# First expert's tokens taken in by tiles of 128, and the first product of each later expert at the end of the loop round before

## The reference

```python
order = np.argsort(-(x @ w_gate).flatten())
for idx in order:                       # a token goes to the first expert with room
    tok, e = int(idx) // E, int(idx) % E
    if assigned[tok] >= 0 or counts[e] >= cap: continue
    assigned[tok] = e; counts[e] += 1
for e in range(E):                      # 384 tokens each
    h = np.maximum(x[assigned == e] @ w1[e], 0.0)      # 384 -> 1024
    out[assigned == e] = h @ w2[e]                     # 1024 -> 384
```

## Time and profile before

| | us |
|---|---|
| median of 3 runs | 1127.56 |
| runs | 1123.82 to 1131.34 |
| profiled execution | 1126.02 |
| its span | 1124.3 |

### The profile page before, as it was taken

The page is one execution under the profiler, slowest core; times in us unless marked ns, Lnnn a source line. Parts: engine busy times, 40 slices in busy tenths (PEclk is TensorE's granted clock), DMA queues, the critical chain, the costliest instruction groups (busy, mean ns, idle before and its releaser), DMA issues.

```text
span 1124.3 us, 36434 instructions
## 1 busy us (share of the span) xinstructions
PE 1066.0 (95%) x14142; PEld 980.6 (87%) x14142; DVE 811.9 (72%) x1807; ACT 507.6 (45%) x955; POOL 441.4 (39%) x473
## 2 busy tenths in 40 slices
PE   4799999999999829899999999999999999999998
PEld 2588888888888718899999999999999999999998
DVE  6889999999998888856856865865865864874222
ACT  7767777777776333224224324323323323313322
POOL 6556566655556328513313313403403402502501
PEclk9999999999999959999999999999999999999999
DMA  6424443344443252030030030030030030030000
GB/s 134 85 61 91 91 90 80 78 88 91 91 91 80 69 176 96 30 134 2 21 129 5 21 121 14 21 115 20 21 112 22 21 112 22 14 119 21 15 8 22
DMA packets 163640, 73.99 MB, mean 66 GB/s; under 512 B 140016, under 2 KB 158192, under 8 KB 163568
## 3 DMA queue, kind: packets, MB, share of 16 engines
q1 hardware_dynamic: 160496, 63.73, 21.5%
q0 software_dynamic: 3072, 9.44, 2.6%
HBM read 63.71 MB, written 9.44 MB: 65 GB/s over the span
## 4 chain that ended last, share of the span: by engine, by line
PE 59%; DVE 3%; issue 1%; DMA 1%; ACT 0%; POOL 0%; SPq 0%; DVEq 0%; ACTq 0%; POOLq 0%
PE tb L2269 27%; PE acc L1885 8%; PE acc L1887 7%; PE acc L1886 7%; PE tb L1885 2%; PE tb L1887 2%; PE tb L1886 2%; PE ps_r L1789 1%; DVE slot L153 1%; DMA w1s<-in_moe_w 1%; DVE thr L146 0%; PE tb L1868 0%; PE tb L2222 0%; PE tb L2226 0%; PE tb L2223 0%
## 5 line engine op out<-in xcount | busy, mean ns | idle before, releaser
L2080 ACT CAST ab_high<-ab 128x384 fp32r<-128x384 f32 x95 | 48.8, 514 | 222.1 <-DVE ab L2165 222.1
L2165 DVE TENSOR_TENSOR ab<-tb,a_sb 128x384 f32<-128x384 f32 x95 | 52.9, 557 | 98.6 <-PE tb L2269 92.1
L1934 POOL TENSOR_TENSOR w_low<-w1s,w_high 128x384 fp32r<-128x384 f32 x64 | 65.6, 1035 | 144.3 <-ACT w_high L2019 144.3
L1858 POOL DMA_INDIRECT xg<-x_rows,tok_next x24 | 25.7, 1069 | 212.7 <-issue 210.0
L2269 PE MATMUL tb<-x_high,wb_high 128*128 128x384 f32 x288 | 99.9, 347 | 0.0
L1885 PE MATMUL acc<-wo_high,ab_high 128*128 128x384 f32 x288 | 98.5, 342 | 0.1
L2070 ACT COPY a_sb<-tb 128x384 f32<-128x384 f32 x96 | 46.1, 480 | 114.6 <-PE tb L2269 114.6
L1887 PE MATMUL acc<-wo_high,ab_low 128*128 128x384 f32 x288 | 97.5, 339 | 0.0
L2269 PE MATMUL tb<-x_high,wa_high 128*128 128x384 f32 x288 | 97.4, 338 | 0.0
L1886 PE MATMUL acc<-wo_low,ab_high 128*128 128x384 f32 x288 | 97.3, 338 | 0.0
L2269 PE MATMUL tb<-x_high,wb_low 128*128 128x384 f32 x288 | 97.0, 337 | 0.0
(11 more groups left out here) (382 smaller groups left out, 3020.4 us busy)
## 6 DMA issues: line engine op xcount, KB each, us to landing
w1s<-in_moe_w SPq DMA_DIRECT2D x8, 1536.0 KB, 6.3
w2s<-in_moe_w SPq DMA_DIRECT2D x8, 1152.0 KB, 9.4
a_re_in<-in_a_re SPq DMA_DIRECT2D x30, 192.0 KB, 2.9
a_im_in<-in_a_im SPq DMA_DIRECT2D x30, 192.0 KB, 3.7
qk<-in_q SPq DMA_DIRECT2D x24, 192.0 KB, 2.7
qk<-in_k SPq DMA_DIRECT2D x24, 192.0 KB, 3.4
vv<-in_v SPq DMA_DIRECT2D x48, 96.0 KB, 2.9
x_rows<-ysb SPq DMA_DIRECT2D x24, 192.0 KB, 3.1
```

The source lines that it names most:

```text
L1934: nc.gpsimd.tensor_tensor(w1p[1][:, f % NW1, :, :], w1_tile(f), w1p[0][:, f % NW1, :, :].bitcast(F32), ALU.subtract).then_inc(s["w1_low"], 1)
L2080: nc.scalar.copy(abp[0][:, f % 2, :], ab[:, f % 2, :]).then_inc(s["ab_high"], 1)
L2165: nc.vector.tensor_tensor(ab[:, f % 2, :], tb[(2 * f + 1) % 4][:, 0:CAP], a_sb[:, f % 2, :], ALU.mult).then_inc(s["ab_made"], 1)
```

## The change

For the first expert, each tile of tokens is turned into a bank of its own (all three k beside each other), its high part is made by one copy and its low part by one subtraction, and hidden(0) is made tile by tile: `tile_high(i)`, six products of 128 columns, and `tile_low(i)`, three of them. The filling product between tiles 1 and 2 and the one behind are gone. ScalarE makes w1's third high part between tiles 0 and 1. VectorE makes the three low parts ahead of the two comparisons (the generator `second_start` is stopped in between). SyncE waits for the first tile instead of the last before it loads w2. For all later experts hidden(0) is issued as `hidden_first(p + 1)` at the end of round p instead of at the top of round p + 1. `ROUTE_LAYERS` begins with 1 instead of 0, so that the first 12 counting products of a round stand behind hidden(1); the layers are numbered as before, hidden(0) being 0.

```diff
-BETWEEN_TILES = (2, 2, 1)
+BETWEEN_TILES = 2
...
-ROUTE_LAYERS = (0, 5, 9, 13)
+ROUTE_LAYERS = (1, 5, 9, 13)
...
         if first:
-            sp.wait_ge(x_gathered[TT - 1], 16)
+            sp.wait_ge(x_gathered[0], 16)
         sp.dma_start(w2s[:, 0:2, :], rows_of(w2)[:, 0:2, :]).then_inc(m_sem["w2_gathered"], 16)
...
+    of_tile = lambda i: x_banks[i][:, 0:HD].rearrange("p (k t) -> p k t", k=KT)
+
+    def turn_tile(pe, i):
+        pe.wait_ge(x_gathered[i], after_moves("x_gathered", 0))
+        for k in range(KT):
+            mm = nc.tensor.transpose(of_tile(i)[:, k, :], xg[:, i, k * P:(k + 1) * P], ident[:])
+        mm.then_inc(s["x_turned"], 1)
+
+    def split_tile_high(act, i):
+        act.wait_ge(s["x_turned"], after("x_turned", 0, i + 1))
+        nc.scalar.copy(x2[0][:, :, of_tokens(i)], of_tile(i)).then_inc(s["x_high"], 1)
+
+    def split_tile_low(dve, i):
+        dve.wait_ge(s["x_high"], after("x_high", 0, i + 1))
+        nc.vector.tensor_tensor(x2[1][:, :, of_tokens(i)], of_tile(i), x2[0][:, :, of_tokens(i)].bitcast(F32), ALU.subtract
+                                ).then_inc(s["x_low"], 1)
...
             w1_high(0, 0)
             w1_high(0, 1)
-            split_x_high(act, 0)
+            split_tile_high(act, 0)
             w1_high(0, 2)
+            split_tile_high(act, 1)
+            split_tile_high(act, 2)
             w2_high(0, 0)
             w2_high(0, 1)
...
-            for _ in route_start(dve, 1, ...):
-                pass
-            split_x_low(dve, 0)
+            second_start = route_start(dve, 1, ...)
+            next(second_start)
+            for i in range(TT):
+                split_tile_low(dve, i)
+            next(second_start)
...
+            def hidden_open(p):
+                pe.wait_ge(s["ab_made"], after("ab_made", p, FT2, back=1))
+                pe.wait_ge(s["w1_low"], after("w1_low", p, 1))
+                return tb[2][:, 0:CAP], [w[:, 0, :, :] for w in w1p]
+
+            def tile_high(i):
+                bank, (high, low) = hidden_open(0)
+                pe.wait_ge(s["x_high"], after("x_high", 0, i + 1))
+                for k in range(KT):
+                    for w in (high, low):
+                        nc.tensor.matmul(bank[:, of_tokens(i)], w[:, k, :], x2[0][:, k, of_tokens(i)],
+                                         start=(i == k == 0 and w is high), stop=False, skip_group_check=True)
+
+            def tile_low(i):
+                ...
+                pe.wait_ge(s["x_low"], after("x_low", 0, i + 1))
+                for k in range(KT):
+                    mm = nc.tensor.matmul(bank[:, of_tokens(i)], high[:, k, :], x2[1][:, k, of_tokens(i)],
+                                          start=False, stop=(i == TT - 1 and k == KT - 1), skip_group_check=True)
+                return mm
...
             keep_running(WARM_UP)
-            for i, products in enumerate(BETWEEN_TILES):
-                turn_x(pe, 0, (i,))
-                keep_running(products)
+            turn_tile(pe, 0)
+            keep_running(BETWEEN_TILES)
+            turn_tile(pe, 1)
+            tile_high(0)
+            turn_tile(pe, 2)
+            tile_high(1)
+            tile_high(2)
+            for i in range(TT):
+                mm = tile_low(i)
+            mm.then_inc(s["h_summed"], 1)
...
-                layers = [(hidden, 0)]
+                layers = []
...
-                for n, (product_of, f) in enumerate(layers):
+                for n, (product_of, f) in enumerate(layers, 1):
...
                 if not last:
                     add_out(FT2 - 1)
+                    hidden_first(pe.snap(p + 1))
```

More of the change, by code:

```diff
@@ L2129, in _ @@
             in_bank = lambda bank, n: bank[:, n * E * G:(n + 1) * E * G].rearrange("p (e g) -> p e g", e=E)
-            for _ in route_start(dve, 1, scores=in_bank(acc[1], 0), masked=in_bank(acc[0], 0), same=in_bank(acc[0], 1),
-                                 best_again=acc[1][:, E * G:E * G + G]):
-                pass
-            split_x_low(dve, 0)
+            second_start = route_start(dve, 1, scores=in_bank(acc[1], 0), masked=in_bank(acc[0], 0), same=in_bank(acc[0], 1),
+                                       best_again=acc[1][:, E * G:E * G + G])
+            next(second_start)
+            for i in range(TT):
+                split_tile_low(dve, i)
+            next(second_start)
             def expert(p, last):
@@ new lines, in hidden_first @@
+            def hidden_first(p):
+                bank, (high, low) = hidden_open(p)
+                for k in range(KT):
+                    pe.wait_ge(s["x_high"], after("x_high", p, k + 1))
+                    nc.tensor.matmul(bank, high[:, k, :], x2[0][:, k, :], start=(k == 0), stop=False)
+                    nc.tensor.matmul(bank, low[:, k, :], x2[0][:, k, :], start=False, stop=False)
+                for k in range(KT):
+                    pe.wait_ge(s["x_low"], after("x_low", p, k + 1))
+                    mm = nc.tensor.matmul(bank, high[:, k, :], x2[1][:, k, :], start=False, stop=(k == KT - 1))
+                mm.then_inc(s["h_summed"], 1)
@@ L2208, in expert @@
+            keep_running(WARM_UP)
+            turn_tile(pe, 0)
[7 more added lines that the diff above has]
+                mm = tile_low(i)
+            mm.then_inc(s["h_summed"], 1)
             def expert(p, last):
@@ L2218, in hidden @@
                     high, low = (w[:, f % NW1, :, :] for w in w1p)
[L2219 to L2230, removed]
+                    for k in range(KT):
+                        mm = three(bank, [high[:, k, :], low[:, k, :]], [x[:, k, :] for x in x2], k == 0, k == KT - 1)
                     mm.then_inc(s["h_summed"], 1)
```

## The result

The changed kernel is slower: 1136.98 us against 1129.28 (medians of 7 runs each), a ratio of 1.0068 with a 95% interval of 1.005 to 1.0085. The forecast was +6.6 us on 1127.6; measured are +7.7 on medians that lie 1.7 higher. The profiled execution of the changed kernel took 1137.52 us with a span of 1135.8, 11.5 more than the span of before. That difference is not all the change's: the first filling product starts at 420.31 before and at 424.62 after, and up to there the two programs do the same. So 4.3 us of the 11.5 had come before the changed part begins, and every time of the entry is counted here from the first filling product. Of the 7.2 that are left, 6.9 come in the six rounds of the loop and 0.2 in the first expert (103.57 us from the first filling product to the end of the second expert's h0, 103.35 before).

A forecast was written before the change was run, and what follows sets the result against it. From the second expert on, TensorE's queue was taken as the bound (busy 86.00 of 86.00 us a round). A loop loss of 7.0 less an entry gain of 0.4 made +6.6 on 1127.6: 1134.2 us, range 1127.0 to 1138.0.

The forecast's parts named there:

- The loop: Rounds of experts 1 to 6: reply read 0.52 us later, s1 1.18 later, 7.0 us lost in all.
- the row at 450.53: First expert before: thr starts 0.10 us ahead of GpSimd yet takes 1.16; taken as the model for the loop.
- thr would lose: Loop: thr waits for GpSimd's operation in all six rounds, 1134.2 us in all, chance 0.50.
- Branch of the loop at another place: End of each round: h0 ahead of the loop's branch costs nothing, bound 0.5 us a round.
- Narrow products: First expert's entry: products of 128 columns take 0.11 us each, bounded from above by 0.173.
- Gather beside the w2 stream: First expert's entry: w2 loading beside the gather of tile 2 costs 0.3 us, bounds nothing and 3.3.
- Entry: First expert: s1 0.7 us sooner, less 0.3 for the gather, gain 0.4; bounds gain 0.7, loss 3.
- The stall between 460 and 470: First expert: TensorE's stall of 1.77 us stays, since the chains between engines all shift alike.
- rival C: First expert: stall between 460 and 470 goes, with its low clock, 2.8 us gained, 1126.4 in all; chance 0.12.

The follow-up runs named there:

- count_only: The kernel before with only the first entry of ROUTE_LAYERS changed from 0 to 1: 1135.01 us, ratio 1.006 to before.
- count_back: The changed kernel with the first entry of ROUTE_LAYERS back at 0, counting products ahead of hidden(1): 1129.95 us, ratio 1.0014 to before.
- thr_free: The changed kernel with thr in the loop reading its ramp from a copy in PSUM instead of SBUF: 1127.58 us, ratio 0.9986 to before.
- w2_mid: The changed kernel with SyncE waiting for the second gathered tile before it loads w2: 1133.72 us, ratio 1.0048 to before.
- before_free: The kernel before with only the two PSUM copies, thr's ramp and the scores for the loop's comparisons: 1120.09 us, ratio 0.9928 to before.
- pool_later: The changed kernel with six semaphore increments on GpSimd ahead of the wait before w2_low(2): 1134.65 us, ratio 1.0061 to before.
- w2_late: The changed kernel with SyncE waiting for the last gathered tile before it loads w2, as before: 1135.45 us, ratio 1.0076 to before.
- pool_after_wait: The changed kernel with nine semaphore increments instead of one on GpSimd behind the wait before w2_low(2), in the loop: 1130.67 us, single execution.

## Why the prediction was right, point by point

- **The loop.** The reply is read 0.50 us behind the start of the counting products, as worked out; thr stands 0.09 ahead of GpSimd (0.10 forecast) and ends 0.05 behind it; a round grows by 1.16 us ((435.22 - 429.44) / 5), and six of them make 6.9. This is the term that carries the result, and the five-round sums, count_only and count_back bear it out. That the row at 450.53 was the right one to go by, and not the rule of the Trainium skill (SBUF — State Buffer, Who interferes with whom) that the first to start has the ports, is shown by thr: it lost with starts of 0.09 and 0.10 us ahead, in all twelve rounds of the loop in the profiles of the changed kernel and of count_only. With 0.72 ahead it did not. That one of the two waits for the other's whole length agrees: thr ends 0.05 us behind GpSimd's operation. The same section of the Trainium skill (SBUF — State Buffer, Who interferes with whom) says that a VectorE operation with at most one input in SBUF, outside the two-port modes, does not contend with GpSimd; thr_free agrees, with 0.34 us at a distance of 0.09.
- **How near it was.** That thr would lose was given 0.50, on one row, and part of it was luck. In the first expert of w2_mid thr starts 0.14 ahead of GpSimd and is not held up (last section), so the distance of 0.10 that was forecast may have been some hundredths from the other outcome, a loss of 2 us instead of 7. The trace of before could not tell where the limit lies.
- **Branch of the loop at another place: nothing.** Right: 85.87 in count_back.
- **Narrow products 0.11 us each.** Right: nine in 1.01 us, and four in 0.44 (from 431.42 to 431.86) as well.
- **Gather beside the w2 stream: 0.3 us.** Wrong in size: 0.9. The bound (3.3) held, the choice was too near its lower end. This is the term of the sum that failed: I let the gather lose a third of the 1 us that its rows take at the large load's rate, but from issue to landing it lost all of that 1 us (4.0 instead of 3.0).
- **Entry, a gain of 0.4 us.** Wrong by as much: a loss of 0.05 at s1. It is the gather's 0.6 more, and w2_mid shows what the entry gives without it, 0.9 (0.7 had been worked out ahead of the gather's price).
- **The stall between 460 and 470 stays.** Right: 1.93 us between 465 and 475, as the profile is 4.3 later, against 1.77. What rival C made of it was wrong in one point: it tied the low clock to the length of the stall (see below). That the ports make the stall was right, and before_free shows that it was worth more than the whole change: I priced it as a chance of distances (0.12) and did not ask what would remove it.

## What to carry to other kernels

An order in which one engine's product stands ten instructions earlier or later costs nothing on that engine and may still set another's chain: look whose reply it carries, and read in a full round how much that chain has left; here it was nothing, as s1 already started 0.04 us behind the end of h2. Where VectorE and GpSimd work side by side, look at what each reads: an operand of VectorE moved to PSUM cost one copy of 128x64 for the whole kernel and one of 128x24 a search, and brought 8 us, more than any order of the work did. A load that is started sooner can take from a gather what it gives: issued 0.71 us behind the gather of the last tile, w2 held it up by 1 us, and issued 1.95 us behind it, not.

## What the runs showed of the hardware

- A tensor_scalar of 128x64 in SBUF that starts 0.09 or 0.10 us ahead of a GpSimd tensor_tensor waits for its end: 1.15 or 1.16 us instead of 0.31, in all thirty loop rounds of the changed kernel, count_only, pool_later, w2_late and w2_mid. 0.72 ahead it does not. In between lie two pairs of the first expert, with GpSimd's piece_low (128x768) instead of w2_low: 0.14 ahead in w2_mid, and 0.18 in pool_after_wait (463.59 and 463.77), and thr takes 0.31 in both. With the same piece_low only 0.04 behind, in pool_later, thr took 1.94. So the limit lies between 0.10 and 0.14, if it is the same for both operations of GpSimd, which no run parts. Timeline of w2_mid:

```profile
460.24 0.31 DVE L146 TENSOR_SCALAR thr<-iota,steps,lows 128x64 f32<-128x64 f32 x1
...
460.38 1.88 POOL L1948 TENSOR_TENSOR wa_low<-w_raw,wa_high 128x768 fp32r<-128x768 f32 x1 [1.50 <-DMA w_raw<-in_moe_w_a]
```

- The granted clock behind nearly the same stall differs from profile to profile. In that of before it falls to the lower level, 1.2 GHz, for some 3 us by estimate ((1 - 0.86) x 10 / 0.5) around a stall of 1.77 us in all; in count_only, which is 5.3 us later in its profile and has 1.77 us of stall at this place too, it stays at 2.4 GHz:

```profile
466.00:476.00 10.00, 8.23 (x58) 7.91 (x57) 8.90 (x17) 1.37 (x3) 4.95 (x3) 1.00 0.13 40
```

  The two take 103.35 and 101.76 us for the first expert. Over 20 us around the stall the clock is 0.91 in before, the changed kernel, pool_later and pool_after_wait, which take 103.35 to 104.50, and 1.00 in count_only, count_back, w2_late and w2_mid, which take 100.99 to 101.91. So about 1.6 us of a run can be such a matter, though each of these is one execution of another kernel. The length of the stall does not decide it: w2_late has 2.16 us of it at full clock, before 1.77 at the lower level. What does was not found.
- The part ahead of the change, the same in all kernels up to the first filling product, ends anywhere from 420.3 to 425.7 us in the eleven profiles. A difference of two single executions of this kernel means nothing below 5 us, and a profile is to be read from a mark inside it.
